# Heads of a pair at rows 0 and 64, and scores in two row tiles straight from the decayed queries

## The reference

```python
for t in range(S):                      # S = 768, D = 48
    state = alpha[:, :, t, :, None] * state + np.einsum('bhd,bhe->bhde', k[:, :, t], v[:, :, t])
    y[:, :, t] = np.einsum('bhd,bhde->bhe', q[:, :, t], state)
```

## Time and profile before

| | us |
|---|---|
| median of 3 runs | 802.44 (799.65 to 802.95) |
| the profiled execution | 802.52 |
| its span, first to last instruction | 800.7 |
| TensorE busy | 757.8 |
| VectorE busy | 467.4 |
| ScalarE busy | 221.8 |

### The profile page before, as it was taken

The page is one execution under the profiler, slowest core; times in us unless marked ns, Lnnn a source line. Parts: engine busy times, 40 slices in busy tenths (PEclk is TensorE's granted clock), DMA queues, the critical chain, the costliest instruction groups (busy, mean ns, idle before and its releaser), DMA issues.

```text
span 800.7 us, 11806 instructions
## 1 busy us (share of the span) xinstructions
PE 757.8 (95%) x4708; PEld 734.6 (92%) x4708; DVE 467.4 (58%) x1015; ACT 221.8 (28%) x414; POOL 75.5 (9%) x123
## 2 busy tenths in 40 slices
PE   5799889999999999999998689999999999999997
PEld 4698889988999889998998589999999999999997
DVE  5786767768775787755674782636354453532121
ACT  2242522234221343123322242122312232122110
POOL 1011100003000120005103211100120010000000
PEclk9699999999999999999999899999999999999999
DMA  7430411322122212207125411200130010000000
GB/s 218 138 121 24 117 43 40 106 64 49 43 77 70 70 41 66 54 30 219 40 76 170 140 50 46 65 1 30 60 89 12 30 59 0 29 0 30 1 30 30
DMA packets 20585, 51.63 MB, mean 64 GB/s; under 512 B 2469, under 2 KB 14777, under 8 KB 20537
## 3 DMA queue, kind: packets, MB, share of 16 engines
q1 hardware_dynamic: 17032, 40.16, 17.0%
q0 software_dynamic: 2816, 9.10, 3.7%
q10 hardware_dynamic: 688, 1.71, 0.7%
HBM read 41.50 MB, written 9.46 MB: 64 GB/s over the span
## 4 chain that ended last, share of the span: by engine, by line
PE 82%; DVE 10%; DMA 3%; ACT 2%; issue 2%; POOL 1%; DVEq 0%
PE bank L1044 65%; PE bank L1068 5%; PE bank L1093 4%; PE bank L1089 3%; DMA decay_k_q<-in_akq 2%; DVE fwd L799 1%; PE bank L1081 1%; DVE rev L785 1%; PE bank L1050 1%; ACT qd L619 1%; PE bank L1224 1%; DVE u_kept L1005 1%; DMA u_new<-x_scratch,mirrored_rows 1%; DVE qu L805 1%; PE bank L1114 1%
## 5 line engine op out<-in xcount | busy, mean ns | idle before, releaser
L1044 PE MATMUL bank<-ut_hi,w_c_parts 128*128 128x384 f32 x576 | 163.6, 339 | 1.3 <-DVE ut_lo L982 1.3
L996 DVE SCALAR_TENSOR_TENSOR hidden_lo<-bank,hidden_hi 128x384 fp32r<-128x384 f32 x96 | 53.3, 556 | 127.4 <-ACT hidden_hi L718 126.4
L1044 PEld LDWEIGHTS bank<-ut_hi,w_c_parts 128*128 128x128 f32 x576 | 105.5, 188 | 1.5 <-issue 1.5
L718 ACT ACTIVATE hidden_hi<-bank 128x384 fp32r<-128x384 f32 x96 | 47.3, 492 | 200.0 <-PE bank L1044 200.0
L1044 PE MATMUL bank<-w_c_hi,hidden_hi 128*128 128x384 f32 x288 | 96.6, 335 | 0.7 <-DVE u_kept L1005 0.7
L1044 PE MATMUL bank<-ut_lo,w_c_parts 128*128 128x384 f32 x288 | 96.4, 335 | 0.0
L1044 PE MATMUL bank<-w_c_hi,hidden_lo 128*128 128x384 f32 x288 | 96.3, 335 | 0.0
L1044 PE MATMUL bank<-w_c_lo,hidden_hi 128*128 128x384 f32 x288 | 96.3, 334 | 0.0
L1044 PE MATMUL bank<-w_sg_hi,vn_hi 128*128 128x384 f32 x192 | 67.7, 353 | 0.7 <-ACT u_gelu L651 0.7
L1044 PE MATMUL bank<-w_sg_lo,vn_hi 128*128 128x384 f32 x192 | 64.8, 338 | 0.0
L1044 PE MATMUL bank<-w_sg_hi,vn_lo 128*128 128x384 f32 x192 | 64.7, 337 | 0.0
(11 more groups left out here) (169 smaller groups left out, 1552.7 us busy)
## 6 DMA issues: line engine op xcount, KB each, us to landing
decay_k_q<-in_akq SPq DMA_DIRECT2D x21, 576.0 KB, 4.8
x_scratch<-x_half SPq DMA_DIRECT2D x8, 579.0 KB, 3.3
out_tiles<-u_kept SPq DMA_DIRECT2D x24, 192.0 KB, 2.0
values<-in_v SPq DMA_DIRECT2D x18, 192.0 KB, 4.7
x_quarters<-x_scratch SPq DMA_DIRECT2D x16, 168.9 KB, 5.4
raw_weights_b<-in_w_second SPq DMA_DIRECT2D x3, 768.0 KB, 4.4
u_new<-x_scratch SPq DMA_DIRECT2D x4, 576.0 KB
decay_k_q_b<-in_akq SPq DMA_DIRECT2D x3, 576.0 KB, 7.0
```

The lines of the kernel that those rows point to most:

```text
L718: nc.scalar.activation(hid[0][:, i % 4, :], HB[i % 2][:, 0:HS], ACT.Relu).then_inc(hhi_done, 1)
L996: nc.vector.scalar_tensor_tensor(out=hid[1][:, i % 4, :], in0=HB[i % 2][:, 0:HS], scalar=0.0, in1=f32(hid[0][:, i % 4, :]), op0=ALU.max, o ...
L1044: ins = nc.tensor.matmul(dst, a, c, start=start and n == 0, stop=stop and n == len(passes) - 1)
```

## The change

A head's 48 rows now begin at row 0 or row 64 (`HR = 64`), and all tiles of the attention have `PR` = 112 rows in place of 96. Rows 48 to 63 hold alpha 1, and k and q 0, filled in when the inputs are laid out. `qd` and its semaphore are gone. The scores of each head are a matmul of their own, 48 rows deep, from `kd` and `qu` directly, and TensorE waits for VectorE's `qk_done`. Head 0's matmuls use the upper half of the array (rows 0 to 63) and write bank `sc[0]`, head 1's use the lower half and write `sc[1]`, so a bank holds the four pairs of one head, and both banks are announced with the last pair. The mask writes to every second 128 columns of `sm`. The transposed keys have 448 columns instead of 384. The other products keep their shapes, but for 112 rows or weight columns where there were 96.

```diff
+HR = 64
+PR = HR + D
...
-                if step == "query":
-                    act.wait_ge(qk_done, i + 1)
-                    for j in range(2):
-                        ins = nc.scalar.activation(bufs["qd"][:, j], bufs["qu"][:], ACT.Copy, scale=blk[:, j:j + 1])
-                    ins.then_inc(qd_done, 1)
                 if step == "scores":
                     act.wait_ge(kt_done, i + 1)
-                    nc.scalar.copy(bufs["kn"][:].rearrange(flat), ky[:, 0:G * PP]).then_inc(kn_done, 1)
+                    nc.scalar.copy(bufs["kn"][:].rearrange(flat), ky[:, 0:G * PR]).then_inc(kn_done, 1)
...
-                        nc.vector.tensor_tensor(sm[:, 2 * x:2 * x + 2].rearrange("p g j t -> p (g j) t"),
-                                                sc[x][:].rearrange("p (a t) -> p a t", a=4),
+                        nc.vector.tensor_tensor(sm[:, :, x, :], sc[x][:].rearrange("p (a t) -> p a t", a=4),
...
-                        ins = nc.tensor.transpose(ky[:, g * PP:(g + 1) * PP], kd[:, g, :], ident[0:PP, 0:PP])
+                        ins = nc.tensor.transpose(ky[:, g * PR:(g + 1) * PR], kd[:, g, :], ident[0:PR, 0:PR])
...
-                    pe.wait_ge(qd_done, i + 1)
+                    pe.wait_ge(qk_done, i + 1)
                     if c > before:
                         pe.wait_ge(st_done, (NT - 1) * n + c - before)
                     for g in range(G):
-                        ins = nc.tensor.matmul(sc[g // 2][:, (g % 2) * 256:(g % 2 + 1) * 256], kd[:, g, :],
-                                               qd[:, :, g, :], start=True, stop=True)
-                        if g % 2:
-                            ins.then_inc(sc_done, 1)
+                        for j in range(2):
+                            at = slice(j * HR, j * HR + D)
+                            ins = nc.tensor.matmul(sc[j][:, g * P:(g + 1) * P], kd[at, g, :], qu[at, g, :], start=True,
+                                                   stop=True)
+                            if g == G - 1:
+                                ins.then_inc(sc_done, 1)
...
-                            ins = nc.tensor.matmul(sc[0][0:PP, g * PP:(g + 1) * PP], kn[:, g, :],
+                            ins = nc.tensor.matmul(sc[0][0:PR, g * PP:(g + 1) * PP], kn[:, g, :],
                                                    values[:, g * PP:(g + 1) * PP], start=True, stop=True)
```

More of the change, by code:

```diff
@@ L170, in build @@
         ve2 = place("ve2", [P, NT], F32, region(24))
[L171 to L174, removed]
+        g_end = place("g_end", [PR, 2, G], F32, region(32))
+        g_blk = place("g_end_by_block", [PR, G, 2], F32, region(32))
+        g_inv = place("g_inv", [PR, G], F32, region(16))
+        blk = place("head_of_row", [PR, 2], F32, region(8))
         warm = place("warm_up", [P, 2], F32, region(8))
         spare = place("spare", [P, 2], F32, region(8))
-        zeros = place("zeros", [PP, P], F32, region(P * 4))
+        zeros = place("zeros", [PR, P], F32, region(P * 4))
         rows = place("mirrored_rows", [P, NI], mybir.dt.uint32, region(NI * 4))
@@ L198, in attention_set @@
         def attention_set(at_raw, at, tag):
-            bufs = {"raw": place("decay_k_q" + tag, [PP, 3, G, P], F32, at_raw)}
-            for name, shape in (("fwd", [PP, G, P]), ("rev", [PP, G, P]), ("kd", [PP, G, P]), ("qu", [PP, G, P]),
-                                ("qd", [PP, 2, G, P]), ("kn", [P, G, PP]), ("sm", [P, G, 2, P])):
+            bufs = {"raw": place("decay_k_q" + tag, [PR, 3, G, P], F32, at_raw)}
+            for name, shape in (("fwd", [PR, G, P]), ("rev", [PR, G, P]), ("kd", [PR, G, P]), ("qu", [PR, G, P]),
+                                ("kn", [P, G, PR]), ("sm", [P, G, 2, P])):
                 bufs[name] = place(name + tag, shape, F32, at)
@@ L208, in build @@
         val = place("values", [P, 2, DM], F32, at_v)
-        st = place("state", [PP, G, PP], F32, at)
-        std = place("state_decayed", [PP, 2, G, PP], F32, at + 4 * G * PP)
+        st = place("state", [PR, G, PP], F32, at)
+        std = place("state_decayed", [PR, 2, G, PP], F32, at + 4 * G * PP)
         set_b, at = attention_set(at_sg, at_sg + 3 * 4 * G * P, "_b")
@@ L293, in build @@
         qk_done = sem("qk_done")
-        qd_done = sem("qd_done")
         kd_done = sem("kd_done")
@@ L808, in attend @@
                     m = (NT - 1) * n + c
-                    nc.vector.tensor_tensor(g_blk[:], g_end[:, c % 2].unsqueeze(2).to_broadcast([PP, G, 2]),
-                                            blk[:].unsqueeze(1).to_broadcast([PP, G, 2]),
+                    nc.vector.tensor_tensor(g_blk[:], g_end[:, c % 2].unsqueeze(2).to_broadcast([PR, G, 2]),
+                                            blk[:].unsqueeze(1).to_broadcast([PR, G, 2]),
                                             ALU.mult).then_inc(g_blk_done, 1)
@@ L815, in attend @@
                                             st[:].rearrange("p g (j d) -> p g j d", j=2),
-                                            g_blk[:].unsqueeze(3).to_broadcast([PP, G, 2, D]),
+                                            g_blk[:].unsqueeze(3).to_broadcast([PR, G, 2, D]),
                                             ALU.mult).then_inc(std_done, 1)
@@ L827, in attend @@
                     dve.wait_ge(kv_done, m + 1)
-                    kv = sc[0][0:PP, 0:G * PP].rearrange("p (g n) -> p g n", g=G)
+                    kv = sc[0][0:PR, 0:G * PP].rearrange("p (g n) -> p g n", g=G)
                     if c == 0:
@@ L1054, in attend @@
                 values = val_first[:, c] if before else val[:, c % 2]
-                kd, qu, qd, kn, sm = (bufs[x] for x in ("kd", "qu", "qd", "kn", "sm"))
+                kd, qu, kn, sm = (bufs[x] for x in ("kd", "qu", "kn", "sm"))
                 if step == "scores":
@@ L1330, with by_chunk @@
     from concourse.bass_utils import run_bass_kernel_spmd
-    def by_chunk(a):
+    def by_chunk(a, rest):
         a = a.reshape(B, G, 2, NT, P, D).transpose(0, 3, 2, 5, 1, 4)
-        return a.reshape(B * NT, PP, G, P)
+        out = np.full((B * NT, PR, G, P), rest, np.float32)
+        for j in range(2):
+            out[:, j * HR:j * HR + D] = a[:, :, j].reshape(B * NT, D, G, P)
+        return out
     def by_rows(w):
         return w.reshape(-1, P, w.shape[1]).transpose(1, 0, 2).reshape(P, -1)
-    akq = np.stack([by_chunk(inputs[name]) for name in ("alpha", "k", "q")], 2)
+    akq = np.stack([by_chunk(inputs[name], rest) for name, rest in (("alpha", 1), ("k", 0), ("q", 0))], 2)
     tab_ch, tab_seq, ident, mask = tables()
     host = {
-        "akq": akq.reshape(B * NT, PP, -1),
+        "akq": akq.reshape(B * NT, PR, -1),
         "v": inputs["v"].transpose(0, 2, 1, 3).reshape(B * NT, P, DM),
@@ L1351 @@
         "tab_ch": tab_ch, "tab_seq": tab_seq, "ident": ident, "mask": mask,
-        "head_of_row": (np.arange(PP)[:, None] // D == np.arange(2)[None, :]).astype(np.float32),
+        "head_of_row": (np.arange(PR)[:, None] // HR == np.arange(2)[None, :]).astype(np.float32),
         "mirrored_rows": mirrored_rows(),
```

## The result

The changed kernel takes **788.78 us** (787.44 to 789.67, 4 runs) where the one before took 802.56 beside it: a ratio of 0.9835, 95% interval 0.9808 to 0.9862. That is 13.8 us less. The forecast was 778, 24.1 us less. Direction and range held; the size was 57% of the forecast.

What follows compares the result with a forecast made beforehand. TensorE was taken to bound the kernel at every stage. Gains of 5.0 us up to 85, 5.0 to 120, then 2.1 and 12.0 to 364 sum to 24.1, taking 802.44 to 778 us; range 771 to 799.

Steps and rivals of the forecast that it cites:

- The likeliest case: Score matmuls of the two row tiles run side by side, weight loads included: 0.90 us per chunk; 778 us, chance 0.50.
- the loads follow each other: Rival at the scores: the two tiles' weight loads run serially, scores 1.81 us per chunk; 796 us, chance 0.20.
- The half rival: Rival at the scores: the two tiles overlap only in part, about half; 787 us, chance 0.12.
- I price a switch at 0 to 0.03, and cost it at nothing: Around each chunk's scores: entering or leaving the row-tiled form takes 0 to 0.03 us, counted as nothing.
- The slower rival: Array drains at each switch, s us twice per chunk, with serial scores; at s = 0.25, 808 us; chance 0.08.
- The prediction's own signs of being wrong: Score starts evenly 0.11 us apart, a gap of 0.15 or more around the scores, or low clock beyond 50 us.
- up to 85 us: Start of the kernel, stepped through: 5.0 us won, from 4.3 to 6.4.
- The third load's own part: At the start, the third chunk's larger load adds its own delay to `rev`; with the first load's 0.5, 0.9 us.
- its lower end: Gain at 84.7 us if TensorE, idle some 4 us near 41 to 45, enters a new low-clock stretch: 4.3 us.
- 85 to 120 us: Two `qd` waits and two chunks' score savings, no clock fall near 113: 5.0 us won.
- From there to the end of the attention: From 120 to 364 us, TensorE-bound: three chunks give 2.1, two batches of waits and six chunks each 12.0.
- The waits: TensorE's idle time ahead of scores after 160 us, 1.9 us in each of two batches, goes: 3.8 us.

Runs made afterwards that it cites:

- the first experiment: Changed kernel with each score matmul over all 112 rows, so no row tiles (heads' scores not kept apart): 798.51 us, ratio 0.9943 to the kernel before.
- the head-by-head kernel: Changed kernel with head 0's four score pairs issued before head 1's four instead of alternating: 797.49 us, ratio 0.9945 to the kernel before.
- the first one with fillers: Changed kernel with 32 filler matmuls (64 for the hardware) ahead of batch 0's first product, loads whole: 793.27 us, ratio 0.9877 to the kernel before.

## Why the prediction was right or wrong

**Right: the tiles run side by side.** The likeliest case had the scores in eight slots of the 128-column filler, 0.90 us. They are eight pairs 0.112 us apart. The rival "the loads follow each other" (1.81) is what the whole-array kernel shows, 1.80, and only there. The half rival is out too, though its 787 lies nearest to the 788.8 measured: the time alone would have picked the wrong mechanism.

**Wrong: "I price a switch at 0 to 0.03, and cost it at nothing".** It costs 0.19 to enter and 0.20 to leave by the starts, 0.38 per chunk by the first experiment. I read it off, where weights of two columns stand between full ones and the spacing does not change. That is another form: few *columns*, but 96 or 97 rows. Nothing in the trace before had matmuls on half of the *rows*, so those rows were no bound. The slower rival had priced a switch at 0.17 to 0.34 from the 0.26 us that a matmul lasts against the 0.09 between starts, and the 0.19 and 0.20 measured lie in it; what was wrong there was to pair it with serial scores. Both mechanisms hold at once, and that case was not on my list. The prediction's own signs of being wrong showed it: a gap of 0.15 or more at the first score and after the last (0.19 and 0.21), and low clock beyond 50 us (until 53). With s = 0.19 and tiles side by side, the forecast's own sum gives 15 times (0.83 less 0.15 less 0.38), 4.5, in place of 10.2; measured 15 times 0.32, 4.8. Over the 24 chunks the switches take some 9 us of TensorE's time (an estimate, 24 times 0.39). That the range held all the same is its width, 28 us, and not the sum.
The Trainium skill ("TensorEngine Tiling (Array Packing)", Key Properties) says that a changed tiling mode drains the engine. The runs here agree as far as a cost at each switch goes, 0.19 and 0.20 us, for which the page gives no price; that it is a drain, no run here shows.

**Wrong: "up to 85 us", 5.0 forecast, nothing measured.** The step that failed is that `rev` of the fifth chunk starts at 39.1 (it was 41.45) and of the third 0.9 later (2.6). For the first load the forecast let only 3 of the 5.1 us grow with the bytes, 0.5; it took 0.9. The third load's own part was put at 0.4 and was 1.7. So the third chunk's scores began at 29.22, where the forecast had 27.45 (its own terms, 27.95 with 0.9 later and 1.34 earlier, give 27.51). The fifth's load was issued 2.65 later (35.05 against 32.40), since VectorE was late from the third on. TensorE then stood idle and ran at 0.50 from 46.4 to 53. The forecast had named that as its lower end, 4.3. A stretch of 6.6 us at half clock costs 3.3, and the fifth `rev` came 2.35 later than forecast; together that is about the 5.1 that are missing, but no run took the two apart. `qd`'s removal moved the weight pieces forward, which did little: with 96 rows and without `qd`, `rev` of the third chunk came at 20.00 against 19.66.

**Right, 85 to 120 us:** 5.0 forecast, 5.3 measured (0.1 behind at 84.8, 5.2 ahead at the scores near 128), with no fall of the clock near 113, as forecast.

**From there to the end of the attention (351.60, before 366.84):** 14.1 forecast, 10.0 measured. The waits gave 4.7 (forecast 3.8), 15 chunks at 0.32 make 4.8 (forecast 10.2), and the last 0.5 is more than a steady chunk's share in the last chunk of each batch, which has no state to update: the very last took 0.50 less than before. k-v products grew by 0.09 (forecast 0.11), transposes by 0.05 (0.04); no TensorE idle time is left, and v_gelu no longer stands behind the query.

**After that** the forecast had nothing, and 1.5 is lost. At 448 the first product of the relu network takes 4.71 us for 18 matmuls at a clock of 0.66 (448 to 453 in the table by stretch); before, the same 18 took 3.14:

```profile
463.35 3.14 PE bank L1044 x18
```

Work ahead of it is the same in both; why the clock fell in one and not in the other was not tested. One trace of each can't tell it from chance: from the last scores to the end, where all 14 kept traces do the same work, they take 441.5 to 444.0 us (442.0 before, 442.9 after).

Sum: −0.1 + 5.3 + 10.0 − 1.5 = 13.7, the difference of the spans. Of the 10.4 that the forecast had too much, 5.4 is the chunks (the switch), 5.1 the start and 1.5 the clock late, less 0.9 of waits, 0.5 of last chunks and 0.3 before 120 that gave more.

## What to carry to other kernels

Price a change into a row-tiled form and out of it at about 0.4 us (measured here with f32, 48 rows and 128 columns at the full clock), and set that against what the tiles save in one run of them: here 0.90 against 0.38, in a run of 8 pairs; with 3 pairs, 0.34, nothing is left. Keep the run unbroken, and alternate the tiles from one matmul to the next. Where two rivals are two mechanisms, ask for the case in which both act, and don't let a row bound an operation whose form it doesn't have.

## What the runs showed of the hardware

An f32 matmul of 48 rows and 128 columns with its own 128-column weight load has a slot of 0.112 us, and two of them in different row tiles share that slot, weight loads included: 16 in 8 slots. This is at sizes where the load sets the pace: 16 matmuls of 48 columns took 1.91 us too.

In the head-by-head kernel the starts read as if matmuls of the second tile began while three of the first's were still to come: the sixth start stands 7 ns after the fifth, the eighth and ninth are as close. The Trainium skill ("TensorE: Matmul & The Clock Gate", Part 3, The mechanism) says that matmuls start in program order without exception. The trace tells them apart: the last matmul of each head raises `sc_done`, and head 0's, the eighth in program order, is the eleventh of the sixteen to start (128.763). So three of head 1's began before it, and the measurement speaks against the rule for this case.

The column of the granted clock can be wrong at the start. In the head-by-head kernel it reads 1.00 from 10 to 47 us:

```profile
10.00:47.00 37.00, 36.34 (x174) 34.22 (x175) 27.34 (x66) 6.02 (x9) 2.54 (x4) 1.00 0.57 176
...
27.92 3.65 PE L1045 MATMUL bank<-causal_mask,ident 128*128 128x128 f32 x16
54.57 1.96 PE L1045 MATMUL bank<-causal_mask,ident 128*128 128x128 f32 x16
```

But the 16 filler matmuls at 27.92 take 3.65 us and the same 16 at 54.57 take 1.96. So it ran at the lower of its two levels until about 47, and 1.00 stands where the trace has no record of the clock: its first record is at 46.9. In the trace before the first is at 14.2, and 16 fillers at 9.59 take 3.68. The mean clocks of these two executions are therefore too high; whether the clock was low at the start is read better from the length of a known group.

How long the low clock lasts at the start also differs between traces that do the same work up to there: the record has it from 22.4 to 29.2 us in the changed kernel and from 24.0 to 41.1 in the first one with fillers, which come later. So what one trace says of the clock at the start is not yet an effect of the change.
